# Batch 0 of an attention and MLP kernel: wide value products, six chunks prepared at once, fillers and Fourier tiles in another order, buffers on 128 bytes

## The chip, the cores and the metric

The kernel runs on one NeuronCore of a Trainium2 chip. The metric is the time of one execution on the device in microseconds (us). Instructions run on five engines, each with its own in-order queue: PE (TensorE, matmuls; PEld is its weight load), DVE (VectorE), ACT (ScalarE), POOL (GpSimd) and SP, which issues most DMAs. The engines wait for each other by semaphores only.

## What is computed

Four batches go through linear attention with a decaying state, then a Fourier mixing block with an MLP, then a token mixing block with an MLP. All is float32; products that need it are made of three fp32r matmuls on high and low parts (`three`).

```python
# attention: B=4, H=8, S=768, D=48
for t in range(S):
    state = alpha[:, :, t, :, None] * state + einsum('bhd,bhe->bhde', k[:, :, t], v[:, :, t])
    y[:, :, t] = einsum('bhd,bhde->bhe', q[:, :, t], state)
x = y of all heads side by side            # 4 x 768 x 384
# first block
u = x + real(fft(fft(x, axis=1), axis=2))
un = (u - mean(u)) / sqrt(var(u) + 1e-6)   # over the 384
x = u + relu(un @ w_ch1) @ w_ch2           # 384 -> 1536 -> 384
# second block
u = x + token_mlp(x)                       # over the 768 tokens, 256 wide
out = u + relu(u @ w2_ch1) @ w2_ch2
```

## The kernel before

**Attention in visits.** Two heads make a unit; a unit has six chunks of 128 tokens, so a batch has 4 units and 24 visits (`STEPS`), one for each chunk k. PE's part of visit k (`visit` under `block.tensor`): the scores of chunk k+1 (`attn_scores`, L1313; the two heads lie on rows 0 to 47 and 64 to 111), keys times values of chunk k+1 (`attn_kv`, L1326, needs `krt` from ACT), the value products of chunk k (`attn_back`, L1335: `at` of one head is the stationary operand and that head's 48 columns of `vt` stream), the product with the decayed state (L1340, 96 columns, not for the first chunk of a unit), and the transpose of the keys of chunk k+2 (`attn_turn`, L1306). An fp32 matmul shows as two instructions in the trace, so the two value products are x4 there. DVE masks the scores (`at`, L977), adds up the state (`st`), and prepares the chunks' decay products by scans (`piece_suffix`, `piece_prefix`, three chunks in one piece in batch 0); POOL multiplies them into keys and queries (`prep_k`, `prep_q`) and decays one head's state (`dec`); ACT copies `krt`, `x`, the other `dec`, and in some visits tests the range of the decays (`tested`, L658) or makes a weight's high part (`weight_hi`, at the visits in `HI_AT`; POOL's low parts, `weight_lo`, are at `LOW_AT`).

**Batch 0 has no MLP beside it.** Its 24 visits run first and alone; the visits of batches 1 to 3 are laid between the MLP matmuls of the batch before (the slots h of `VISIT`). After the visits comes the tail of slots h = 31 to 47 (`tail` on each engine, an order written by hand): fold and flips, the six Fourier tiles `f1` (L1299 to L1301 by way of `three`, each wants the low part `xl` of its tile from DVE, and its result is split to `gh` by ACT and `gl` by DVE), the second Fourier products `f2_v`, `f2_u`, `f2_middle`, their sums on DVE and POOL, the normalisation, three transposes (`norm`), and then the first MLP stage. For batch 0 `fill(n)` puts n matmuls on constants, whose result nobody reads, behind the visits and behind the slots named in `FILL`.

**The first MLP slots.** DVE's last slot of the tail (h = 47) reduces the range of the next batch's first unit (`extreme`, L826) and prepares its first chunk (`prep`), and then comes the rest of the normalisation of batch 0 (`norm_stats`, L1081, `norm_var`, `norm_scale`), on which ACT's `std` and `norm_rows` wait, and behind them in ACT's queue the copy `qz` for the first scores of batch 1 (L1317).

**Loads.** SP loads the units in order; POOL issues the four table loads in visits 3 to 6. Buffers lie one behind the other from byte 16512 (a multiple of 128); by this `hh` and `hl`, the stationary operands of the second MLP product, begin 64 bytes past a multiple of 128, `nh`, `nl`, `u2h` and `u2l`, the streamed operands of the first, at a multiple.

## Time and profile before

| | |
|---|---|
| median of 3 runs | 927.83 us (927.74 to 928.92) |
| the profiled execution | 927.87 us, its span 926.1 us |
| PE busy | 904.9 us, 98% |
| DVE, ACT, POOL busy | 49%, 33%, 22% |
| batch 0: visits, then tail up to the first MLP matmul | to 71.0 us, to 98.9 us |
| last long wait of PE ends | 107.58 us |

The page gives busy time as the share of the span, and a line PEclk with the clock that TensorE was granted in 40 slices of 23 us, in tenths of 2.4 GHz (5 is 1.2 GHz). Views of the trace give the same by stretches, and the instructions in order of time.

### The profile page before, as it was taken

The numbers are of one execution on the slowest core, as the hardware profiler recorded it, in microseconds if no ns is written. First come the engines' busy times: TensorE is split into PE (matmuls) and PEld (weight loads), VectorE is DVE, ScalarE is ACT, GpSimd is POOL, SyncE is SP. The second block draws the span as 40 slices with busy tenths as digits, with TensorE's granted clock in tenths as the row PEclk, the third lists the DMA queues.
The fourth block names the chain that finished last, engine by engine and source line by source line (L and its number), as shares of the span: only waits on it lengthen the run. The fifth ranks groups of instructions, "written<-read, shape, count | busy, mean of one in ns | idle before, by whom it ended". The sixth has DMA issues, their size and how long they took to land.

```text
span 926.1 us, 14520 instructions
## 1 busy us (share of the span) xinstructions
PE 904.9 (98%) x5378; PEld 871.6 (94%) x5378; DVE 451.8 (49%) x1078; ACT 303.7 (33%) x794; POOL 201.4 (22%) x330
## 2 busy tenths in 40 slices
PE   8999799999999999999999999999999999999998
PEld 6888699999899998999999999999999999999998
DVE  5446777756877658777472226221422232223121
ACT  3445445432555424444323333211122122112111
POOL 4443463302333103333013332000200020002000
PEclk8559899999999999999999999999999999999999
DMA  9802122004031040220017102000200020000000
GB/s 272 323 1 76 41 60 58 27 6 111 27 86 32 27 116 26 60 58 27 2 69 230 52 3 95 6 26 1 76 0 25 0 76 0 25 10 16 0 25 26
DMA packets 14360, 50.87 MB, mean 55 GB/s; under 512 B 1408, under 2 KB 5632, under 8 KB 12368
## 3 DMA queue, kind: packets, MB, share of 16 engines
q1 hardware_dynamic: 13728, 47.01, 16.3%
q0 software_dynamic: 576, 3.15, 0.9%
q8 instruction: 31, 0.51, 0.2%
q14 instruction: 25, 0.20, 0.1%
HBM read 40.72 MB, written 9.44 MB: 54 GB/s over the span
## 4 chain that ended last, share of the span: by engine, by line
PE 90%; DVE 5%; ACT 2%; DMA 1%; issue 1%; SPq 0%; DVEq 0%; ACTq 0%
PE bank L1299 13%; PE bank L1301 13%; PE bank L1300 13%; PE pair L1299 11%; PE pair L1300 11%; PE pair L1301 11%; PE bank L1335 5%; PE pair L1317 4%; PE bank L1340 3%; PE pair L1326 2%; PE pair L1313 2%; DMA vt<-v 1%; PE bank L1306 1%; PE bank L1434 1%; DVE stats L1081 1%
## 5 line engine op out<-in xcount | busy, mean ns | idle before, releaser
L1168 DVE SCALAR_TENSOR_TENSOR hl<-bank,hh 128x384 fp32r<-128x384 f32 x192 | 106.9, 557 | 333.5 <-ACT hh L742 333.5
L742 ACT ACTIVATE hh<-bank 128x384 fp32r<-128x384 f32 x192 | 94.2, 491 | 353.2 <-PE bank L1301 353.0
L1299 PE MATMUL bank<-nh,w1h 128*128 128x384 f32 x288 | 102.3, 355 | 0.4 <-DVE nl L1124 0.4
L1299 PE MATMUL pair<-w2h,hh 128*128 128x384 f32 x288 | 101.6, 353 | 0.0
L1299 PE MATMUL bank<-u2h,w3h 128*128 128x384 f32 x288 | 97.2, 338 | 0.8 <-DVE u2l L1255 0.8
L1299 PE MATMUL pair<-w4h,hh 128*128 128x384 f32 x288 | 98.0, 340 | 0.0
L1300 PE MATMUL pair<-w4l,hh 128*128 128x384 f32 x288 | 97.3, 338 | 0.0
L1301 PE MATMUL bank<-nh,w1l 128*128 128x384 f32 x288 | 97.3, 338 | 0.0
L1301 PE MATMUL pair<-w4h,hl 128*128 128x384 f32 x288 | 97.2, 338 | 0.0
L1300 PE MATMUL bank<-nl,w1h 128*128 128x384 f32 x288 | 97.1, 337 | 0.0
L1300 PE MATMUL pair<-w2l,hh 128*128 128x384 f32 x288 | 97.0, 337 | 0.0
L1301 PE MATMUL pair<-w2h,hl 128*128 128x384 f32 x288 | 97.0, 337 | 0.0
L1301 PE MATMUL bank<-u2h,w3l 128*128 128x384 f32 x288 | 96.6, 335 | 0.0
L1300 PE MATMUL bank<-u2l,w3h 128*128 128x384 f32 x288 | 96.4, 335 | 0.0
L608 POOL TENSOR_TENSOR u<-u,x2l 128x384 f32<-128x384 f32 x24 | 23.6, 1012 | 276.7 <-DVE u L1276 276.7
L525 POOL TENSOR_TENSOR qkap<-qkap,suf 112x128 f32<-112x128 f32 (+1 forms) x81 | 39.8, 491 | 134.5 <-DVE suf L850 121.0
L977 DVE TENSOR_TENSOR at<-pair,mask 128x256 f32<-128x256 f32 x96 | 40.1, 417 | 52.1 <-PE pair L1326 44.1
L1335 PE MATMUL bank<-vt,at 128*128 128x48 f32 x384 | 63.8, 295 | 0.0
L1335 PEld LDWEIGHTS bank<-vt,at 128*128 128x128 f32 x384 | 61.1, 223 | 1.6 <-issue 0.9
L632 ACT ACTIVATE qz<-qkap 48x128 f32<-48x128 f32 x144 | 44.3, 308 | 40.5 <-POOL qkap L533 34.1
L1299 PEld LDWEIGHTS bank<-nh,w1h 128*128 128x128 f32 x288 | 54.8, 190 | 1.4 <-issue 0.8
L1299 PEld LDWEIGHTS bank<-u2h,w3h 128*128 128x128 f32 x288 | 54.1, 188 | 2.1 <-issue 2.1
(189 smaller groups left out, 1886.3 us busy)
## 6 DMA issues: line engine op xcount, KB each, us to landing
qkap<-qka SPq DMA_DIRECT2D x15, 1011.5 KB, 6.5
vt<-v SPq DMA_DIRECT2D x16, 288.0 KB, 7.8
raw_a<-w_ch SPq DMA_DIRECT2D x6, 768.0 KB, 9.1
mid<-u SPq DMA_DIRECT2D x8, 576.0 KB, 2.8
raw_b<-w_ch SPq DMA_DIRECT2D x6, 768.0 KB, 6.0
out<-u SPq DMA_DIRECT2D x8, 576.0 KB, 2.8
xr<-mid SPq DMA_DIRECT2D x7, 576.0 KB, 3.9
raw_t<-w_tok SPq DMA_DIRECT2D x2, 768.0 KB, 5.5
```

The costliest lines, as they stand in the source:

```text
L525: pool.tensor_tensor(keys.rearrange("p (c n) -> p c n", n=P), keys.rearrange("p (c n) -> p c n", n=P), after.rearrange("p (c n) -> p c n", ...
L608: pool.tensor_tensor(u2[:, t, :], u2[:, t, :], x2l[:, t, :].bitcast(F32), ALU.add).then_inc(s_u2, 1)
L632: act.activation(qz[head_rows(h), k % 2, h, :], q_of(a, k, head_rows(h)), ACT.Copy).then_inc(s_qz, 1)
L742: act.activation(hh[:, s % 4, :], bank[s % 2][:, 0:HALF], ACT.Relu).then_inc(s_hhi, 1)
L977: dve.tensor_tensor(at[:, k % 2, :, :], scores, mask[:, None, :].to_broadcast([P, 2, P]), ALU.mult).then_inc(s_at, 1)
L1168: dve.scalar_tensor_tensor(out=hl[:, s % 4, :], in0=bank[s % 2][:, 0:HALF], scalar=0.0, in1=hh[:, s % 4, :].bitcast(F32), op0=ALU.max, op1 ...
L1299: pe.matmul(out_ap, wh, rh, start=first, stop=False)
L1300: pe.matmul(out_ap, wh, rl, start=False, stop=False)
L1301: return pe.matmul(out_ap, wl, rh, start=False, stop=last)
L1317: return pe.matmul(score_bank(a, k)[:, 0:2 * P], k_of(a, k), qz[0:PR, k % 2, :, :].rearrange("p h t -> p (h t)"), start=True, stop=True)
L1335: mm = pe.matmul(y[:, h * D:(h + 1) * D], at[:, k % 2, h, :], vb[:, c, h * D:(h + 1) * D], start=h == 0, stop=c == 0 and h == 1)
L1340: mm = pe.matmul(y, q_of(a, k), dec[0:PR, k % 3, :], start=False, stop=True)
```

## The change

**Value products.** For batch 0 each of the two value products of a visit streams all 96 columns of `vt` (both heads) and writes two groups of 48 columns: the head's own into `y`, which now begins at column 64, and the other head's, of no use, 112 columns away, into columns that nobody reads.

**Preparation.** DVE and POOL prepare chunks 1 to 5 in the visit -2, where chunks 3 to 5 had been spread over the visits -1 and 0.

**Orders.** Fillers: 2 in place of 4 behind the visits, none at slots 31 and 45. The Fourier tiles of the second part run as 1, 2, 0 (`f1_tile`), and `f2_v(0)` waits for five split tiles in place of six, `f2_u(0)` for the sixth. POOL issues the tables in visits 7 to 10; high and low weight parts come two and three visits later; `weight_lo` 7 goes from the end of the tail into batch 1's visits. The early sums of the fold move to the last two visits, in all batches. DVE prepares the next batch's first chunk in slots 45 and 46, between the splits of the normalised tiles, instead of slot 47; the third of these tiles is transposed into another bank and waits no more for the first's split.

**Buffers.** Two sizes are rounded up and three places moved to 128 bytes. By the offsets `hh` and `hl` go from 64 past a multiple of 128 to a multiple (so do `krt`, `at` and `qz`), `nh`, `nl`, `u2h`, `u2l` and `un` from a multiple to 64 past it.

```diff
+ASIDE = 112
...
-KV_AT, T_AT = 384, 256
+KV_AT, T_AT, Y_AT = 384, 256, 64
...
-FILL = {31: 5, 42: 3, 44: 2, 45: 1, 46: 2}
-HI_AT = (9, 11, 13, 15, 17, 19)
+FILL = {42: 3, 44: 2, 46: 2}
+TABLES_AT = 7
+HI_AT = (11, 13, 15, 17, 19, 21)
 HI_FOLD = 9
-LOW_AT = (12, 15, 18)
+LOW_AT = (15, 18, 21)
 LOW_F1 = 6
-LATE_LOW_AT = (0, 2, 4, 6)
+LATE_LOW_AT = (-2, 0, 2, 4, 6)
...
+NEXT_AT = 45
...
+def f1_tile(i):
+    return i % KT if i < KT else (i + 1) % KT
...
+    def aligned(n):
+        return -(-n // P) * P
+    QB = aligned(QW * 4)
...
+    o = aligned(o)
     suf = sb("suf", [P, 2, 3 * HW + 5], o); o += 2 * (3 * HW + 5) * 4
-    krt = sb("krt", [P, 2, PR], o); o += 2 * PR * 4
+    o = aligned(o)
+    krt = sb("krt", [P, 2, P], o); o += 2 * P * 4
...
-    o += 2 * QB
-    o_u = o
+    o = o_u = aligned(o + 2 * QB)
...
-    NORM_BANKS = (6, 7, 6, 6, 6, 6)
+    def norm_bank(b, t):
+        return bank[4 if b == 0 and t == 2 else 7 if t == 1 else 6]
...
-        return visit_bank(a, k)[:, 0:PW]
+        first = 0 if a else Y_AT
+        return visit_bank(a, k)[:, first:first + PW]
...
-                    prep_k(0, 1, 2)
-                    prep_q(0, 1, 2)
-                elif k == -1:
-                    prep_k(0, 3, 3)
-                elif k == 0:
-                    prep_q(0, 3, 3)
+                    for first, n in ((1, 2), (3, 3)):
+                        prep_k(0, first, n)
+                        prep_q(0, first, n)
                 elif k % 3 == 1 and k + 5 < STEPS:
                     prep_k(0, k + 5, 3)
-                elif k % 3 == 2 and k + 4 < STEPS:
+                elif k % 3 == 2 and 0 < k < STEPS - 4:
...
-                if 3 <= k < 7:
-                    pool.dma_start(tables[k - 3][0][:], tables[k - 3][1].bitcast(F32R)).then_inc(s_table, 16)
+                if TABLES_AT <= k < TABLES_AT + 4:
+                    table, source = tables[k - TABLES_AT]
+                    pool.dma_start(table[:], source.bitcast(F32R)).then_inc(s_table, 16)
...
-                if a == 0:
-                    pool.wait_ge(s_un[0], 2)
-                    for i in range(LOW_F1, 2 * NA - len(LATE_LOW_AT)):
-                        weight_lo(i)
                 if a + 1 < B:
-                    prep(a + 1, 0)
+                    prep_k(a + 1, 0, 1)
+                    if a == 0:
+                        weight_lo(LOW_F1)
+                    prep_q(a + 1, 0, 1)
...
-                    piece_suffix(1)
-                    piece_prefix(1)
-                elif k == -1:
-                    piece_suffix(2)
-                elif k == 0:
-                    piece_prefix(2)
-                elif k % 3 == 1 and k + 5 < STEPS:
+                    for i in (1, 2):
+                        piece_suffix(i)
+                        piece_prefix(i)
+                elif k % 3 == 1 and k > 0 and k + 5 < STEPS:
                     piece_suffix(piece_of(k + 5))
-                elif k % 3 == 2 and k + 4 < STEPS:
+                elif k % 3 == 2 and 0 < k < STEPS - 4:
...
-                if k in (FLAG + 2, FLAG + 3):
-                    early_sum(a, k - FLAG - 2)
+                if k in (STEPS - 2, STEPS - 1):
+                    early_sum(a, k - STEPS + 2)
...
+                if h == NEXT_AT and a + 1 < B:
+                    prep_suffix(a + 1, 0)
+                    prep_inverse(a + 1, 0)
+                if h == NEXT_AT + 1 and a + 1 < B:
+                    extreme(a + 1, 0, 0)
                 for t in NORM_AT.get(h, ()):
                     norm_split(a, t)
+                if h == NEXT_AT + 1 and a + 1 < B:
+                    extreme(a + 1, 0, 1)
+                    prep_prefix(a + 1, 0)
                 if h == 46:
                     for i in range(2):
                         fourier_u(a, 4, 2, i)
-                if h == SLOTS - 1 and a + 1 < B:
-                    for i in range(2):
-                        extreme(a + 1, 0, i)
-                    prep(a + 1, 0)
...
+                    if a:
+                        mm = pe.matmul(y[:, h * D:(h + 1) * D], at[:, k % 2, h, :], vb[:, c, h * D:(h + 1) * D],
+                                       start=h == 0, stop=c == 0 and h == 1)
+                    else:
+                        first = Y_AT * (1 - h)
+                        both = visit_bank(0, k)[:, first:first + 2 * ASIDE].rearrange("p (g n) -> p g n", g=2)[:, :, 0:D]
+                        mm = pe.matmul(both, at[:, k % 2, h, :], vb[:, c, :], start=h == 0, stop=c == 0 and h == 1)
...
-                    pe.wait_ge(s_glo, (a + 1) * (2 * KT))
+                    pe.wait_ge(s_glo, a * (2 * KT) + 2 * KT - 1)
...
-                if j == 1:
+                if j == 0:
+                    pe.wait_ge(s_glo, (a + 1) * (2 * KT))
+                elif j == 1:
...
-                elif t == 2:
+                elif t == 2 and b:
                     pe.wait_ge(s_nlo, b * NC + 1)
-                else:
+                elif t > 2:
...
-            fill(4)
+            fill(2)
```

On PE, the visits of chunks 2 and 3 of batch 0 (`at` the masked scores, `vt` the values, `dec` the decayed state, `krt` the turned keys). Before:

```order
L1313 MATMUL pair1<-qkap0_57 128x128 x2
L1326 MATMUL pair1<-vt0_62,krt_70 112x96
L1335 MATMUL bank6<-vt0_62,at_71 128x48 x2
L1340 MATMUL bank6<-dec_74,qkap0_57 128x96
L1306 MATMUL bank6<-ident_97,qkap0_57 128x112
```

Now:

```order
L1330 MATMUL pair1<-qkap0_57 128x128 x2
L1343 MATMUL pair1<-vt0_62,krt_70 112x96
L1358 MATMUL bank6<-vt0_62,at_71 128x2x48 x2
L1362 MATMUL bank6<-dec_74,qkap0_57 128x96
L1323 MATMUL bank6<-ident_97,qkap0_57 128x112
```

Nothing moves here; the third row streams 2x48 columns where it streamed 48.

On PE, the end of batch 0's visits and the start of its tail (`mask`, `ident` are the fillers, `x`, `flip` the flips, `dfth` the first Fourier tile). Before:

```order
L1335 MATMUL bank7<-vt3_93,at_71 128x48 x2
L1340 MATMUL bank7<-dec_74,qkap3_84 128x96
L1487 MATMUL bank0<-mask_96,ident_97 128x256 x4
L1379 MATMUL pair0<-x_64,flip_98 128x384 x2
L1379 MATMUL pair1<-x_64,flip_98 128x384
L1487 MATMUL bank0<-mask_96,ident_97 128x256 x5
L1299 MATMUL pair1<-dfth_53,xh_61 128x194
```

Now:

```order
L1358 MATMUL bank7<-vt3_93,at_71 128x2x48 x2
L1362 MATMUL bank7<-dec_74,qkap3_84 128x96
L1511 MATMUL bank0<-mask_96,ident_97 128x256 x2
L1401 MATMUL pair0<-x_64,flip_98 128x384 x2
L1401 MATMUL pair1<-x_64,flip_98 128x384
L1316 MATMUL pair1<-dfth_53,xh_61 128x194
```

Two fillers ahead of the flips and all five between the flips and the first tile are gone.

On DVE, slots 43 to 47 of batch 0's tail and what follows (`un` normalised rows, `nl` their low parts, `ext`, `suf`, `inv` and the last `qkap0` the next batch's first unit, `stats` the rest of the normalisation). Before:

```order
L1118 TENSOR_SCALAR un_77<-u0_89,mv_103,nrm_104 128x384 x2
L1124 TENSOR_TENSOR nl_86<-bank6,nh_85 128x3x128
L1124 TENSOR_TENSOR nl_86<-bank7,nh_85 128x3x128
L1124 TENSOR_TENSOR nl_86<-bank6,nh_85 128x3x128
L1067 TENSOR_TENSOR u0_89<-u0_89,pair1 128x2x193
L1067 TENSOR_TENSOR u0_89<-u0_89,pair1 128x2x191
L826 TENSOR_REDUCE ext_105<-qkap0_57 112x1 x2
L850 SCALAR_TENSOR_TENSOR suf_69<-qkap0_57,zeros_99 112x128
L856 RECIPROCAL inv_75<-suf_69 112x1
L862 SCALAR_TENSOR_TENSOR qkap0_57<-qkap0_57,inv_75,zeros_99 112x128
L1081 BN_STATS stats_102<-u0_89 128x6 x3
```

Now:

```order
L1131 TENSOR_SCALAR un_77<-u0_89,mv_103,nrm_104 128x384 x2
L865 SCALAR_TENSOR_TENSOR suf_69<-qkap0_57,zeros_99 112x128
L871 RECIPROCAL inv_75<-suf_69 112x1
L1137 TENSOR_TENSOR nl_86<-bank6,nh_85 128x3x128
L1137 TENSOR_TENSOR nl_86<-bank7,nh_85 128x3x128
L839 TENSOR_REDUCE ext_105<-qkap0_57 112x1
L1137 TENSOR_TENSOR nl_86<-pair1,nh_85 128x3x128
L839 TENSOR_REDUCE ext_105<-qkap0_57 112x1
L877 SCALAR_TENSOR_TENSOR qkap0_57<-qkap0_57,inv_75,zeros_99 112x128
L1080 TENSOR_TENSOR u0_89<-u0_89,pair1 128x2x193
L1080 TENSOR_TENSOR u0_89<-u0_89,pair1 128x2x191
```

The two reductions, the two scans and the reciprocal stood between the last sum of `u0` and `stats`; they stand ahead of that sum now, two of them ahead of the splits `nl`.

## Rows read from the trace of the kernel before

**Rows 1.** The page: the span, and the clock granted in 40 slices.

```profile
span 926.1 us, 14520 instructions
PEclk8559899999999999999999999999999999999999
```

**Rows 2.** Stretches: length, busy time (instructions) of each engine, granted clock, DMA share, GB/s.

```profile
14.00:16.00 2.00, 1.21 (x9) 1.04 (x10) 1.20 (x2) 1.89 (x6) 1.31 (x3) 0.92 1.00 306
...
72.00:74.00 2.00, 2.00 (x7) 1.61 (x6) 2.00 (x6) 1.90 (x4) 0.00 (x0) 0.58 0.06 16
...
110.00:112.00 2.00, 2.00 (x9) 1.97 (x9) 0.85 (x3) 0.25 (x2) 1.29 (x3) 0.69 0.00 0
```

**Rows 3.** In order of time: start, us, engine, line, count, idle before and releaser.

```profile
14.06 0.94 ACT L658 ACTIVATE tested<-qkap,limits 112x768 f32<-112x768 f32 x1 [1.74 <-DMA vt<-v]
...
14.18 0.49 PE L1313 MATMUL pair<-qkap 48*128 48x128 f32 x4 [1.32 <-POOL qkap L533]
...
15.29 0.44 PE L1326 MATMUL pair<-vt,krt 128*112 128x96 f32 x2 [0.61 <-ACT krt L625]
```

**Rows 4.** In order of time, PE: scores that open visits, at either clock.

```profile
9.89 0.49 PE L1313 MATMUL pair<-qkap 48*128 48x128 f32 x4
...
11.20 0.49 PE L1313 MATMUL pair<-qkap 48*128 48x128 f32 x4
...
24.95 0.80 PE L1313 MATMUL pair<-qkap 48*128 48x128 f32 x4
...
27.28 0.80 PE L1313 MATMUL pair<-qkap 48*128 48x128 f32 x4
```

**Rows 5.** In order of time, PE: 48 and 96 columns and the next, at either clock.

```profile
11.89 0.60 PE L1335 MATMUL bank<-vt,at 128*128 128x48 f32 x4
...
12.33 0.43 PE L1340 MATMUL bank<-dec,qkap 112*128 112x96 f32 x2
...
12.60 0.26 PE L1306 MATMUL bank<-ident,qkap 112*128 112x112 f32 x1
...
31.30 0.98 PE L1335 MATMUL bank<-vt,at 128*128 128x48 f32 x4
...
32.09 0.71 PE L1340 MATMUL bank<-dec,qkap 112*128 112x96 f32 x2
...
32.58 0.39 PE L1306 MATMUL bank<-ident,qkap 112*128 112x112 f32 x1
```

**Rows 6.** Stretch of six visits at the lower clock, columns as in rows 2.

```profile
47.91:63.78 15.87, 15.87 (x76) 13.15 (x75) 7.00 (x20) 8.40 (x23) 8.29 (x10) 0.50 0.00 0
```

**Rows 7.** In order of time: fillers, low parts, first Fourier tile, first second-stage product.

```profile
70.98 3.26 PE L1487 MATMUL bank<-mask,ident 128*128 128x256 f32 x8
...
75.13 1.49 DVE L1039 TENSOR_TENSOR xl<-xf,xh 128x384 fp32r<-128x384 f32 x3
...
77.98 0.44 PE L1299 MATMUL pair<-dfth,xh 128*128 128x194 f32 x1
...
86.29 0.36 PE L1299 MATMUL pair<-csh,gh 128*128 128x194 f32 x1 [0.82 <-DVE gl L1044]
```

**Rows 8.** In order of time: DVE's splits and reductions, PE's wait for batch 1.

```profile
96.46 1.06 DVE L1124 TENSOR_TENSOR nl<-bank,nh 128x384 fp32r<-128x384 f32 x2 [0.84 <-ACT nh L715]
...
98.18 0.56 DVE L1124 TENSOR_TENSOR nl<-bank,nh 128x384 fp32r<-128x384 f32 x1 [0.66 <-ACT nh L715]
...
99.58 1.80 DVE L826 TENSOR_REDUCE ext<-qkap 112x1 f32<-112x768 f32 x2
...
107.58 1.22 PE L1317 MATMUL pair<-qz,qkap 112*128 112x256 f32 x2 [4.65 <-ACT qz L632]
```

**Rows 9.** In order of time, PE in the second MLP: either product's first matmuls.

```profile
640.36 0.34 PE L1299 MATMUL bank<-u2h,w3h 128*128 128x384 f32 x1
...
641.92 0.34 PE L1299 MATMUL pair<-w4h,hh 128*128 128x384 f32 x1
...
643.51 0.34 PE L1299 MATMUL bank<-u2h,w3h 128*128 128x384 f32 x1
```

More of the change, by code:

```diff
@@ L100, in program @@
     XB = NC * DM * 4
-    QB = QW * 4
+    def aligned(n):
+        return -(-n // P) * P
+    QB = aligned(QW * 4)
     o_q = o
@@ L369, in f1_out @@
     def f1_out(i):
-        cols = f1_cols(i // KT, i % KT)
+        cols = f1_cols(i // KT, f1_tile(i))
         out_ap = bank[5 + i % 3][:, 0:cols.stop - cols.start]
-        return out_ap.rearrange("p (a n) -> p a n", a=2) if i % KT == 1 else out_ap
+        return out_ap.rearrange("p (a n) -> p a n", a=2) if f1_tile(i) == 1 else out_ap
     def v_terms(a, j):
@@ L624, in attn_krt @@
                     act.wait_ge(s_vis, visited(a, k - 2))
-                    act.activation(krt[:, s % 2, :], turned(a, k), ACT.Copy).then_inc(s_krt, 1)
+                    act.activation(krt[:, s % 2, 0:PR], turned(a, k), ACT.Copy).then_inc(s_krt, 1)
             def attn_qz(a, k, h):
@@ L678, in split_x @@
                 act.wait_ge(s_fold, a * 7 + (4, 7)[part])
-                for t in range(KT):
+                for i in range(part * KT, (part + 1) * KT):
+                    t = f1_tile(i)
                     m = slice(t * P, (t + 1) * P)
@@ L687, in split_g @@
                     act.wait_ge(s_fold, a * 7 + 7)
-                act.activation(g_slot(gh, i // KT, i % KT), f1_out(i), ACT.Copy).then_inc(s_ghi, 1)
+                act.activation(g_slot(gh, i // KT, f1_tile(i)), f1_out(i), ACT.Copy).then_inc(s_ghi, 1)
             def copy_v(a, j):
@@ L715, in norm_split @@
                 act.activation(nh[:, :, t * P:(t + 1) * P],
-                               bank[NORM_BANKS[t]][:, 0:DM].rearrange("p (k n) -> p k n", k=KT), ACT.Copy
+                               norm_bank(b, t)[:, 0:DM].rearrange("p (k n) -> p k n", k=KT), ACT.Copy
                                ).then_inc(s_nhi, 1)
@@ L845, in prep_suffix @@
                 slot, first = suf_at(k)
+                if k % NC == 0:
+                    dve.wait_ge(*unit_loaded(a, k // NC))
                 if k >= RING:
@@ L1035, in split_x @@
             def split_x(a, part):
-                for t in range(KT):
-                    dve.wait_ge(s_xhi, a * 6 + 3 * part + t + 1)
+                for i in range(part * KT, (part + 1) * KT):
+                    t = f1_tile(i)
+                    dve.wait_ge(s_xhi, a * 6 + i + 1)
                     m, r = slice(t * P, (t + 1) * P), slice(part * KT, (part + 1) * KT)
@@ L1043, in split_g @@
                 dve.wait_ge(s_ghi, a * (2 * KT) + i + 1)
-                dve.tensor_tensor(g_slot(gl, i // KT, i % KT), f1_out(i), g_slot(gh, i // KT, i % KT).bitcast(F32),
+                dve.tensor_tensor(g_slot(gl, i // KT, f1_tile(i)), f1_out(i), g_slot(gh, i // KT, f1_tile(i)).bitcast(F32),
                                   ALU.subtract).then_inc(s_glo, 1)
@@ L1123, in norm_split @@
                 cols = slice(t * P, (t + 1) * P)
-                dve.tensor_tensor(nl[:, :, cols], bank[NORM_BANKS[t]][:, 0:DM].rearrange("p (k n) -> p k n", k=KT),
+                dve.tensor_tensor(nl[:, :, cols], norm_bank(b, t)[:, 0:DM].rearrange("p (k n) -> p k n", k=KT),
                                   nh[:, :, cols].bitcast(F32), ALU.subtract).then_inc(s_nlo, 1)
@@ L1325, in attn_kv @@
                 pe.wait_ge(s_krt, s + 1)
-                return pe.matmul(kv_of(a, k), krt[:, s % 2, :], vt[unit_buffer(a, k // NC)][:, k % NC, :], start=True,
+                return pe.matmul(kv_of(a, k), krt[:, s % 2, 0:PR], vt[unit_buffer(a, k // NC)][:, k % NC, :], start=True,
                                  stop=True)
@@ L1334, in attn_back @@
                 for h in range(2):
-                    mm = pe.matmul(y[:, h * D:(h + 1) * D], at[:, k % 2, h, :], vb[:, c, h * D:(h + 1) * D],
-                                   start=h == 0, stop=c == 0 and h == 1)
+                    if a:
[5 more added lines that the diff above has]
+                        mm = pe.matmul(both, at[:, k % 2, h, :], vb[:, c, :], start=h == 0, stop=c == 0 and h == 1)
                 if c:
@@ L1381, in f1 @@
             def f1(a, i):
-                part, t = i // KT, i % KT
+                part, t = i // KT, f1_tile(i)
                 pe.wait_ge(s_xlo, a * 6 + i + 1)
@@ L1433, in norm @@
                 for k in range(KT):
-                    mm = pe.transpose(bank[NORM_BANKS[t]][:, k * P:(k + 1) * P], un[:, t % 3, k * P:(k + 1) * P],
+                    mm = pe.transpose(norm_bank(b, t)[:, k * P:(k + 1) * P], un[:, t % 3, k * P:(k + 1) * P],
                                       ident[:, :])
```

## The prediction

> **What bounds the kernel now.** I read the page first: PE is busy 98% of the span, so on the face of it only PE's work counts. The clock line tells otherwise for the start [rows 1]: 0.5 in two slices of 23 us where everything after is near full. The stretches [rows 2] show when: the clock falls at the end of the slice 14 to 16, in which PE had little to do, and comes back in the slice 72 to 74. In between lie the visits of batch 0: PE is never idle there and runs at 1.2 GHz. Such "busy" time is not work that must take so long. Two visits of the same make (first chunk of a unit, no state product) give the ratio: 9.89 to 11.20 at 2.4 GHz, 24.95 to 27.28 at 1.2 GHz, 1.31 against 2.33 us, 0.562 [rows 4]. What the engine did ahead of the two returns: a run of 256-column fillers from 70.98 on [rows 7], and MLP matmuls in the slice 110 to 112, which shows 0.69 [rows 2]. Ahead of the fall: waits [rows 3]. The change can win in three places: the visits (15.3 to 71.0), the tail up to batch 1's first scores (71.0 to 107.6), and the rate of the matmuls themselves.
>
> My sum is made against the profiled execution, 927.87 us (span 926.1 and 1.8 around it); the median of the runs is 927.83, so nothing is to be converted. About 0.2% (1.9 us) is what a measurement of this kernel can tell from no change.
>
> **Six chunks at once: nothing by itself.** PE's wait for POOL's queries at 14.18 (1.32 us) goes [rows 3]. But what is late next is the same event: ACT's range test of unit 1 stands in visit 0 as before, waits for unit 1's load until 14.06, takes 0.94, and `krt` behind it lets PE go on at 15.29 [rows 3]. SP's order, and so the landing, is untouched. PE then does the scores of chunk 3 early and waits some 1.9 us for `krt` in place of 1.3 and 0.6. The scans that DVE now does ahead of the first `at`, and POOL's two products ahead of the first `dec`, lie in time in which both waited for PE; 0 each, at most 0.3. I expect the clock to fall here again.
>
> **Wide value products: the term that decides.** Each of the four instructions of a visit streams 96 columns in place of 48, which makes a visit more like the stretches before the two returns. If the clock comes back in the visits, each visit after that shrinks. What the columns cost: four 48-column instructions take 11.89 to 12.33, 0.11 each, two of 96 columns 12.33 to 12.60, 0.135 each; at the lower level 31.30 to 32.09, 0.197, and 32.09 to 32.58, 0.245 [rows 5]. So +0.10 us a visit at the higher level and +0.19 at the lower; ends 0 (the weight load hides it) and the price of the rival D below. The Trainium skill (TensorE: Matmul & The Clock Gate, Part 2, "LDWEIGHTS") makes a load of 128 columns take 107 ns whatever is streamed, which the 0.11 agrees with and the 0.135 does not; by it the wide products would be free and the forecast about 2 us lower.
>
> Remaining visits: 22 value products from 15.3 to 71.0, 55.7 us, 2.53 each. At the higher level 2.53 x 0.562 = 1.42, +0.10 = 1.52. The other engines don't shrink with PE: six visits take 7.00 us of DVE, 8.40 of ACT, 8.29 of POOL [rows 6], 1.17, 1.40 and 1.38 a visit. All fit, but ACT's 0.94 of a range test [rows 3] comes in one piece in 8 visits and keeps `krt` waiting; 8 x 0.94 / 22 = 0.34 at most, 0 at least; I take 0.13, since ACT idles in most visits. So 1.65 a visit, 0.652 of now (1.52 to 1.86). At the lower level 2.72, 1.075 of now.
>
> When does the clock return? No row shows it for such visits. The fillers that begin at 70.98 brought it back before 74 [rows 2, 7]; I allow about twice that, 7 us at the lower level after 15.3. Then 7 / 1.075 = 6.5 of the 55.7 us are done, 49.2 x 0.652 = 32.1 are left, the visits end at 54.4: **-16.6**. Ends inside this case: no fall at all and 1.52 a visit, -22.2; 1.86 a visit, -12.5.
>
> **Loads and weight parts: 0.** Tables two to four visits later, high and low parts two and three visits later: with shorter visits these come at about the clock times of now or before the flips, which wait for the tables. The low part that moves into batch 1 is needed by the first second-stage product of the MLP, several us later.
>
> **Fillers and Fourier tiles: -2.8.** The low parts of the first tile are done at 75.13 + 1.49 / 3 = 75.6, yet the first Fourier matmul runs at 77.98, behind the five fillers [rows 7]: 2.3 us. The order 1, 2, 0 and the earlier start of `f2_v(0)` take the wait of 0.82 before it away [rows 7], since the last tile runs while the one before is split. DVE's queue between them gives back some 0.3. What is late next is the same chain through `gl`, only earlier. If a missing filler lets the clock fall in the tail, up to 2 us come back.
>
> **Next batch's preparation: -1.2.** DVE's reductions (1.80) with scans and reciprocal stand between the last split and the rest of the normalisation, on which ACT's `qz` and so PE's wait of 4.65 hang [rows 8]. Moved forward, they fill DVE's waits of 0.84 and 0.66 for ACT [rows 8], 1.5 us; one reduction ahead of the third split holds the first MLP matmul up by 0.3. Queued behind them are only the sums of `u0`, which come later anyway. The early sums, now in the last two visits, have DVE's free time there: 0, at most +0.3.
>
> **Buffers: -3.0.** In the second MLP nine matmuls with `w3h` as weights take 640.36 to 641.92, 0.1733 each, nine with `hh` 641.92 to 643.51, 0.1767 [rows 9]. `hh` and `hl` begin 64 bytes off and are aligned now. There are 6 x 288 = 1728 such matmuls in both MLPs: 5.7 us if the offset is all of it, 0 if it is something else; and as `nh` and `u2h` move the other way, the same 5.7 could be lost on the streamed side. I take -3.0, nearer to the gain, as the row shows the weight side only.
>
> **Sum:** -16.6 - 2.8 - 1.2 - 3.0 = -23.6; 927.87 - 23.6 = 904.3, say **904**.
>
> **The rivals.**
>
> A, the forecast: the clock returns early in the visits and stays. 904; ends -22.2 - 5 - 5.7 and -12.5 - 2.8, so 895 to 912.
>
> B, it returns halfway or falls again at a wait. With a return at 43 us: 27.7 / 1.075 = 25.8 done, 29.9 x 0.652 = 19.5 left, end 62.5, -8.5; with -7.0 of the rest, 912 (909 to 918). For it: no stretch with visits alone, in 55 us, brought the clock back.
>
> C, the change doesn't do what it adds columns for: the visits stay at 1.2 GHz. 55.7 x 0.075 = +4.2; the tail begins low and without fillers, so the flips and the first tile lose about 1.3 of the gain there: -1.5 - 1.2 - 3.0. 927.87 - 1.5 = 926.4 (923 to 929). For it the same as for B, against it that the fillers, which do nothing but stream more columns, brought it back at once.
>
> D, slower: the product's result is written in two runs of 48 columns with a gap, and the write, not the weight load, sets its pace. Place: L1335, at the lower level. Price: twice the spacing, 0.197 x 4 = 0.79 a visit, 17.4 us over 22 visits, less 5.7 of the rest, 939.6; it decides from 5.7 / 22 = 0.26 a visit on; in the middle 934 (929 to 940). The rows speak neither way, as no matmul of before writes in two runs. The Trainium skill (Advanced Engine Details and Errata, "PSUM Cachelines") says that a non-contiguous pattern in PSUM slows matmuls significantly; no row here shows it, and here the runs are long.
>
> **How the numbers follow.** A 0.58, B 0.15, C 0.14, D 0.10, and 0.03 for a time below A. The point is A's, 904. The range 896 to 927 holds nearly all of A and B and most of C, some 0.82. Faster by over 0.2% (under 926.0): A, B, the 0.03 and a third of C, 0.81. Within: 0.09 of C. Slower: D, 0.10.
>
> **What would show it.** The clock line: one low slice, not two, and the visits ending near 54 us. If it is up before 25 us, A; if only at 40, B; if at the fillers, C. Value products: spacing of 0.13 at the higher level; 0.2 or more speaks for D. `krt` waits for the range test at 15.3 as now. The first Fourier matmul comes 4.6 us behind the last state product, not 7; `f2_v(0)` without a wait; PE's wait for `qz` near 3.5 us. Matmuls with `hh` at 0.174 and those with `u2h` no slower. The prediction is wrong if the clock falls again after each load or range test, or if ACT holds the visits above 1.9 us.

## The result and the profile after

The changed kernel takes 921.81 us (median of four executions, 921.35 to 922.73), the kernel before beside it 928.04: a ratio of 0.9933 (95%: 0.9915 to 0.995). That is 6 us faster where 24 were forecast. An execution of this kernel has one of two times, by whether the clock holds in batch 0's visits; where a kernel showed both, they are told apart below.

The page after, span and clock:

```profile
span 919.5 us, 14499 instructions
...
PEclk8558999999999999999999999999999999999999
```

Two low slices are there as in [rows 1]. The stretches (columns as in rows 2) date them:

```profile
14.00:16.00 2.00, 0.09 (x1) 0.09 (x1) 0.96 (x1) 1.32 (x4) 0.27 (x1) 1.00 1.00 264
16.00:18.00 2.00, 2.00 (x11) 1.75 (x11) 1.30 (x4) 1.36 (x4) 1.08 (x2) 0.50 0.94 244
72.00:74.00 2.00, 2.00 (x7) 1.64 (x6) 1.52 (x5) 1.73 (x4) 0.00 (x0) 0.50 0.03 8
74.00:76.00 2.00, 2.00 (x6) 0.86 (x5) 2.00 (x7) 1.76 (x4) 0.00 (x0) 1.00 0.03 8
```

PE does almost nothing from 14 to 16, the clock is at 1.2 GHz from 16 on, and the visits never bring it back: it is up again from 74 on, behind the fillers that begin at 72.02, as before. The rows that answer to [rows 3], in order of time, show the wait ahead of the fall in one piece now:

```profile
12.94 0.49 PE L1330 MATMUL pair<-qkap 48*128 48x128 f32 x4
...
14.68 0.94 ACT L670 ACTIVATE tested<-qkap,limits 112x768 f32<-112x768 f32 x1 [2.44 <-DMA vt<-v]
...
15.91 0.65 PE L1343 MATMUL pair<-vt,krt 128*112 128x96 f32 x2 [2.49 <-ACT krt L637]
```

One visit at the lower clock, PE in order of time (for rows 4 and 5; the view ends within the last row, of which only the start is read):

```profile
23.02 0.80 PE L1330 MATMUL pair<-qkap 48*128 48x128 f32 x4
...
24.23 1.06 PE L1358 MATMUL bank<-vt,at 128*128 128x96 f32 x4
25.08 0.63 PE L1362 MATMUL bank<-dec,qkap 112*128 112x96 f32 x2
25.51 0.39 PE L1323 MATMUL bank<-ident,qkap 112*128 112x112 f32 x1
25.84 0.58 PE L1330 MATMUL pair<-qkap 48*128 48x128 f32 x2
```

The tail and the way to batch 1, in order of time (for rows 7 and 8):

```profile
72.02 1.97 PE L1511 MATMUL bank<-mask,ident 128*128 128x256 f32 x4
...
76.78 0.36 PE L1316 MATMUL pair<-dfth,xh 128*128 128x194 f32 x1 [0.78 <-DVE xl L1052]
...
84.32 0.36 PE L1316 MATMUL pair<-csh,gh 128*128 128x194 f32 x1
...
104.31 0.84 PE L1334 MATMUL pair<-qz,qkap 112*128 112x256 f32 x2 [3.83 <-ACT qz L644]
```

With the same rows of before (70.98, 77.98, 86.29, 107.58 and the span) they divide the 6.6 us of the two spans:

| stretch | before | after | difference | forecast |
|---|---|---|---|---|
| start to the fillers behind the visits | 70.98 | 72.02 | +1.0 | -16.6 |
| to the first Fourier tile | 7.00 | 4.76 | -2.2 | -2.3 |
| to the first second-stage product | 8.31 | 7.54 | -0.8 | -0.5 |
| to batch 1's first scores | 21.29 | 19.99 | -1.3 | -1.2 |
| to the end of the span | 818.5 | 815.2 | -3.3 | -3.0 |
| sum | | | -6.6 | -23.6 |

One term is wrong, and it is the one that was to decide. Of its +1.0, 0.6 is the later end of the wait (15.91 for 15.29).

Not all of the last row is the buffers' (their own run is below). From the first matmul of the second block to the end the changed kernel is 2.2 us faster. The other 1.1 lie between batch 1's scores and that block, 450.3 us for 451.4, and are not steady: in a second trace of the changed kernel it is 451.1 there. That the row comes near its forecast is in part luck.

### The profile page after: what moved, and what is told of

Read it like the earlier page. It is cut to its first block, busy times and chain, and to the rows that moved or that the text cites. A ratio compares the mean times of both kernels' runs of the same rounds, so it can differ in the third digit from the quotient of the medians.

```text
span 919.5 us, 14499 instructions
## 1 busy us (share of the span) xinstructions
PE 899.2 (98%) x5362; PEld 866.5 (94%) x5362; DVE 453.9 (49%) x1078; ACT 303.7 (33%) x794; POOL 196.1 (21%) x330
## 4 chain that ended last, share of the span: by engine, by line
PE 89%; DVE 6%; ACT 2%; issue 1%; DMA 1%; SPq 0%; DVEq 0%; ACTq 0%
PE bank L1316 13%; PE bank L1317 13%; PE bank L1318 13%; PE pair L1316 12%; PE pair L1317 11%; PE pair L1318 11%; PE pair L1334 4%; PE bank L1353 3%; PE bank L1362 3%; PE pair L1343 2%; PE bank L1358 2%; PE pair L1330 2%; DMA vt<-v 1%; PE bank L1323 1%; PE bank L1458 1%
## 5 line engine op out<-in xcount | busy, mean ns | idle before, releaser
L620 POOL TENSOR_TENSOR u<-u,x2l 128x384 f32<-128x384 f32 x24 | 23.6, 1016 | 275.0 <-DVE u L1293 275.0
L1317 PEld LDWEIGHTS bank<-nl,w1h 128*128 128x128 f32 x288 | 54.7, 190 | 0.4
L1316 PEld LDWEIGHTS pair<-w2h,hh 128*128 128x128 f32 x288 | 54.4, 189 | 0.2
```

Of the source, the lines that this page charges most:

```text
L620: pool.tensor_tensor(u2[:, t, :], u2[:, t, :], x2l[:, t, :].bitcast(F32), ALU.add).then_inc(s_u2, 1)
L1316: pe.matmul(out_ap, wh, rh, start=first, stop=False)
L1317: pe.matmul(out_ap, wh, rl, start=False, stop=False)
```

## The experiments

All are edits of the changed kernel, unless another is named, and were run beside the kernel before.

### Narrow value products: the columns cost nothing

```diff
-                    if a:
+                    if True:
                         mm = pe.matmul(y[:, h * D:(h + 1) * D], at[:, k % 2, h, :], vb[:, c, h * D:(h + 1) * D],
```

> The changed kernel with the value products of batch 0 narrow again (48 columns, the head's own). Theory 1, the wide columns neither cost nor bring anything, since at the lower clock the weight load sets the pace of 48 and of 96 columns alike: value products again 0.21 apart or a little less (the kernel before has 0.20), visits end at 72.0 give or take 0.5, time 921.8 within 1 us. Theory 2, my forecast's price (0.19 us a visit at the lower clock) is right and something else paid it back: the visits end some 4 us earlier and the time is 918. Theory 3, the wide products help in a way not yet seen: 924 or more.

920.9 us (920.2 to 921.6; ratio 0.9908, 0.9891 to 0.9924), with the same two low slices. A visit at the lower clock and the end of the visits, PE in order of time (the view of the visit ends within its last row):

```profile
22.51 0.80 PE L1330 MATMUL pair<-qkap 48*128 48x128 f32 x4
...
23.72 0.98 PE L1353 MATMUL bank<-vt,at 128*128 128x48 f32 x4
24.50 0.71 PE L1362 MATMUL bank<-dec,qkap 112*128 112x96 f32 x2
25.00 0.39 PE L1323 MATMUL bank<-ident,qkap 112*128 112x112 f32 x1
25.32 0.59 PE L1330 MATMUL pair<-qkap 48*128 48x128 f32 x2
```

```profile
71.35 1.97 PE L1511 MATMUL bank<-mask,ident 128*128 128x256 f32 x4
```

From scores to scores it is 2.81 us, with wide products 2.82. Four narrow products take 0.78 and the two that follow 0.50; four wide ones 0.85 and 0.43: 1.28 either way. From the end of the wait to the fillers it is 55.99 us (15.36 to 71.35), with wide products 56.11 (15.91 to 72.02). Theory 1 holds; at this clock the wide columns neither cost nor bring more than 0.1 us.

### Fillers in the wait: the fall was the wait's

```diff
                     mm = attn_scores(a, k + 1)
+                    if a == 0 and k == 2:
+                        for _ in range(6):
+                            pe.matmul(pairs[(k + 1) % 2][:, 0, P:P + 256], ident[:, :],
+                                      mask[:, None, :].to_broadcast([P, 256 // P, P]), start=True, stop=True)
                     if has_state(k + 1):
```

> The changed kernel with six fp32 fillers of 256 columns on PE in the wait of 2.49 us ahead of the fourth keys-times-values product (13.4 to 15.9), about 0.39 us each, so nothing is added to the path. Theory 1, the wait alone makes the clock fall, and a clock that is up stays up in the visits: no low slice before the tail, 56.1 us of visits shrink to 0.56 to 0.65 of it, the visits end near 50, time 897 to 903. Theory 2, the visits themselves hold too little work for the clock: it falls some us later, the visits end at 66 to 72, time 915 to 922. The fillers cost at most 0.5 if they outlast the wait.

900.9 us (900.05 to 902.6; ratio 0.9694, 0.9676 to 0.9712). The page:

```profile
PEclk9998999999999999999999999999999999999999
```

and PE around the place, in order of time:

```profile
13.30 0.49 PE L1330 MATMUL pair<-qkap 48*128 48x128 f32 x4
13.72 2.86 PE L1378 MATMUL pair<-mask,ident 128*128 128x256 f32 x12
16.41 0.34 PE L1343 MATMUL pair<-vt,krt 128*112 128x96 f32 x2
...
48.99 1.06 PE L1515 MATMUL bank<-mask,ident 128*128 128x256 f32 x4
```

The twelve instructions fill the wait, no low slice is left ahead of the tail, and the visits end at 48.99 instead of 72.02. Six matmuls whose result nobody reads are worth 21 us: theory 1, in this place. A wait alone does not always do it: in the tail of the changed kernel PE waited 1.40 us up to 97.03, and the clock shows 1.00 from 94 to 104.

### The same with narrow products: what the wide ones are good for

The two edits above together. 

> The changed kernel with the six fillers in the wait and with narrow value products, beside the same with wide ones. Theory 1 (the wait alone makes the clock fall): as with wide ones, 896 to 903, the narrow ones 0 to 2 us faster as they stream less. Theory 2, wide products are what keeps a clock that is up from falling: with narrow ones it falls again in the visits, time 912 to 922, while with wide ones it stays up.

901.2, 901.4, 906.1 and 909.8 us. The last is the profiled one; its stretches:

```profile
34.00:36.00 2.00, 1.82 (x16) 1.50 (x15) 1.49 (x3) 1.93 (x7) 1.44 (x3) 0.89 1.06 407
36.00:38.00 2.00, 2.00 (x12) 1.75 (x11) 1.81 (x5) 1.16 (x3) 1.33 (x2) 0.50 1.03 390
```

With PE busy 1.8 of 2.0 us the clock fell at about 35.6 all the same. Just ahead PE waited twice for `krt`, 0.21 and 0.18 us (up to 33.70 and 35.50); the wide kernel has the same two waits, 0.22 and 0.18, and does not fall. The result is between the theories: narrow visits hold the clock in some executions only.

### Fillers in batch 1's first wait too

```diff
+                    if a == 1 and k == -1:
+                        for _ in range(10):
+                            pe.matmul(bank[5][:, 0:2 * P], ident[:, :], mask[:, None, :].to_broadcast([P, 2, P]),
+                                      start=True, stop=True)
                     mm = attn_scores(a, k + 1)
```

With wide products: 

> The six fillers in the first wait, and ten more of 256 columns (0.39 us each at the higher clock) in the wait of 3.83 us for batch 1's first scores, so that the second fall of the clock goes too. What runs at the lower clock there takes 5.2 us (83.2 to 88.4) and should take about 3.1: theory, 2 us less than with the first fillers alone, 898 to 900. Rival: the fillers outlast the wait or the clock falls anyway, 901 to 903.

With narrow ones: 

> Both groups of fillers, with narrow value products. With narrow products two of four runs lay at 901.3 and two at 906 and 910, the profiled one with a clock that fell in the visits at 35.6. Theory, wide products give the visits what they lack to hold the clock in every run: narrow again spread from 899 to 908 with a median above that of wide ones, and the wide ones within 2 us of each other. Rival, that spread was chance: both 898 to 901.

Wide 899.0 us (898.4 to 900.1; ratio 0.9678, 0.9653 to 0.9703), narrow 898.5, 899.3, 905.7 and 905.8. PE in the wide kernel, in order of time:

```profile
80.18 4.49 PE L1377 MATMUL pair<-mask,ident 128*128 128x256 f32 x20
84.52 0.60 PE L1334 MATMUL pair<-qz,qkap 112*128 112x256 f32 x2
```

Batch 1's first scores take 0.60 where they took 1.22 in [rows 8] and in the kernel with the first fillers alone: the second fall is gone, 2 us. And the spread of the narrow kernel comes again: of eight narrow executions four kept the clock through the visits, of eight wide ones all, and of four more below. If the columns made no difference, all four losses would fall among the eight narrow ones of these twenty about once in 70. So the wide columns, which did not raise the clock, help to keep it up; the evidence for that is this count.

### Fillers in the fallen visits

The six fillers in visit 6 (`k == 6`) in place of 2. 

> The changed kernel with the six fillers not in the wait but in visit 6, well after the clock has fallen, where nothing waits for them to pass: at the lower clock they add 4.7 us (0.39 us each doubled). Theory 1, wide visits can't raise the clock but hold it once it is up: low from 16 to about 31, then up to the end of the visits, 17 visits at 1.55 to 1.65 in place of 2.5 to 2.8, visits end at 57 to 61, time 907 to 911. Theory 2, the visits lose it again or the fillers don't raise it: visits end at 72 to 77, time 920 to 927.

905.7 us (two executions, 905.4 and 906.1; ratio 0.9753, 0.972 to 0.9785). Stretches:

```profile
20.00:22.00 2.00, 2.00 (x11) 1.52 (x11) 0.24 (x2) 1.42 (x4) 0.95 (x1) 0.50 1.05 337
...
24.00:26.00 2.00, 2.00 (x7) 1.64 (x6) 0.00 (x0) 1.16 (x3) 0.56 (x1) 0.50 1.00 318
26.00:28.00 2.00, 2.00 (x9) 1.67 (x8) 0.00 (x0) 0.00 (x0) 0.00 (x0) 0.74 0.67 270
28.00:30.00 2.00, 2.00 (x18) 1.71 (x17) 0.85 (x3) 0.73 (x3) 0.40 (x1) 1.00 0.79 221
...
46.00:48.00 2.00, 2.00 (x18) 1.43 (x16) 1.69 (x5) 1.67 (x6) 1.85 (x3) 1.00 0.00 0
```

Wide visits at 1.2 GHz stay there though PE shows 2.00 busy of 2.00 (20 to 22); the clock rises at 27, within the fillers (23.99 to 28.2); the visits behind them hold it. The first wait had no fillers here; it was 0.90 us, and the clock fell behind it, at 16.8. The expectation's theory 1, and 1 to 6 us better than its number.

### The work behind the load one visit later

```diff
-RANGE_AT = {0: (1, 0), 1: (1, 1), ...
+RANGE_AT = {1: (1, 0), 2: (1, 1), ...
...
+                elif k in (2, 3):
+                    (piece_suffix, piece_prefix)[k - 2](3)
```

and the same two visits for POOL's `prep_k` and `prep_q`. 

> The changed kernel without fillers, but with the work that waits for unit 1's load one visit later: ACT's two range tests of unit 1 in the visits 1 and 2, DVE's scans and POOL's products for the chunks 6 to 8 in the visits 2 and 3. The wait of 2.49 us for the fourth krt goes; by the landing of the load (14.68) and the lengths of one test, one scan and one product (0.94, 0.96, 0.95) I expect a wait of some 1.2 us one visit later and one of about 1 us at the scores of chunk 6. Theory 1, it is the length of one wait that makes the clock fall: it stays up, no low slice in the visits, time 899 to 906. Theory 2, waits of this size are enough: it falls between 16 and 22, time 917 to 923. In between (some runs one, some the other): it stands near its limit.

916.9 us (916.4 to 917.5; ratio 0.9871, 0.9845 to 0.9897). PE's wait, and the stretches around it:

```profile
19.01 0.49 PE L1334 MATMUL pair<-qkap 48*128 48x128 f32 x4 [1.16 <-POOL qkap L548]
```

```profile
16.00:18.00 2.00, 1.85 (x16) 1.44 (x14) 1.68 (x5) 1.47 (x5) 1.13 (x3) 1.00 1.05 314
18.00:20.00 2.00, 0.99 (x9) 0.90 (x10) 1.15 (x3) 1.31 (x4) 1.74 (x2) 1.00 0.98 301
20.00:22.00 2.00, 2.00 (x12) 1.52 (x11) 1.54 (x4) 0.88 (x4) 0.82 (x3) 0.52 0.95 267
```

The wait of 2.49 went, one of 1.16 came later, and the clock fell behind that one, in all four executions: theory 2. What it gains, 5 us beside the first set of the changed kernel and 3 beside the second (below), are two to three visits more at the full clock and the shorter wait.

### The other parts undone

The tail of before (fillers 4, 5 and 1; tile order 0, 1, 2; `f2_v(0)` behind all six tiles):

> The changed kernel with the tail of the kernel before: fillers 4 behind the visits and 5 and 1 at the slots 31 and 45, Fourier tiles in the order 0, 1, 2 and the first second-stage product behind all six split tiles. In the changed kernel the first Fourier tile comes 4.76 us and the first second-stage product 12.30 us behind the end of the last state product's start (72.02). My forecast was 2.3 for the fillers and 0.8 less 0.3 for the order: with both undone the first tile comes 2.0 to 2.4 us later, the second stage a further 0.5 to 0.8, time 924.0 to 925.0. Rival: the fillers shorten a low stretch, so that the old ones cost nothing: 922.

The next batch's preparation back in DVE's slot 47:

> The changed kernel with the next batch's preparation on DVE back in slot 47, behind the last sum. Theory, as forecast (1.2 us): PE's wait for batch 1's scores goes from 3.83 to 5.0 to 5.4 us, the three batches that follow lose 0.2 to 0.4 each at the same place, time 923 to 924.3. Rival, the move only puts the wait elsewhere (the third split came 1.40 us late in the changed kernel, 0.40 in the kernel before): the first MLP product comes 0.9 earlier, the scores 0.3 to 0.5 later, time within 0.5 of 921.8.

The chunks 3 to 5 in the visits -1 and 0 again:

> The changed kernel with the chunks 3 to 5 prepared in the visits -1 and 0 again. Theory, nothing by itself, as forecast: PE waits for POOL's queries and then for krt as in the kernel before, up to the same landing of unit 1, the clock falls at about 16, time 921.8 within 0.7. Rival: the wait is then in two pieces with some work between them and the visits end up to 1 us earlier or later.

The old tail: 923.4, 924.7 and 926.1 us, and 900.4, 901.3 and 901.3 in the three other executions. Old preparation: seven executions from 924.0 to 928.6, four from 902.5 to 903.2. Old chunks: 919.3 (919.1 to 922.8), never lower. PE's waits in the profiled executions, all of which lost the clock, are the next three fences. Old tail:

```profile
14.40 0.43 PE L1343 MATMUL pair<-vt,krt 128*112 128x96 f32 x2 [1.38 <-ACT krt L637]
```

Old preparation:

```profile
14.36 0.43 PE L1339 MATMUL pair<-vt,krt 128*112 128x96 f32 x2 [1.46 <-ACT krt L637]
...
104.57 1.22 PE L1330 MATMUL pair<-qz,qkap 112*128 112x256 f32 x2 [6.38 <-ACT qz L644]
```

Old chunks:

```profile
14.82 0.49 PE L1336 MATMUL pair<-qkap 48*128 48x128 f32 x4 [1.33 <-POOL qkap L548]
```

In the old tail the first Fourier tile comes 7.73 us behind the start of the last state product (69.46 to 77.19), in the changed kernel 5.18 (71.60 to 76.78): 2.55 for the fillers. From there to the second stage it is 8.32 against 7.54: 0.78 for the order. The old preparation makes the wait for `qz` 6.38 in place of 3.83, a loss of 2.5, more than I expected; from the second Fourier stage to batch 1's scores it is 22.26 us against 19.99. The old chunks change nothing that the landing of unit 1 doesn't. That landing varies: ACT's first test of unit 1 starts between 13.13 and 15.48 us in the traces here, and PE's wait goes with it. With the same landing (test at 13.13) the visits end at 70.04 with the old chunks, and at 70.03 with the new ones in the kernel with the old preparation. The 919.3 is below the 921.1 to 922.5 that I expected, but so is the second set of the changed kernel (below).

### The buffers alone

The kernel before with the changed sizes and places:

> The kernel before with only the buffers of the change (two sizes rounded up, three places on 128 bytes). Theory 1, the 64 bytes of the stationary operands cost 0.0015 us in each of 1728 matmuls: 3 us less than before, 925, mostly in the second MLP, 2.2 to 2.7 us between its first and its last matmul. Rival, the rate has another cause: 928 within 0.5.

926.1 us (924.9 to 927.8; ratio 0.9961, 0.9942 to 0.9981), span 923.2. From the first matmul of the second block to the end of the span it is 365.0 us; in the kernel before 367.1 (from 558.98), after 364.9 (from 554.59). The row of the kernel with the buffers alone:

```profile
558.18 0.44 PE L1303 MATMUL bank<-x2h,t1h 128*128 128x384 f32 x1
```

So 2.1 of its 2.9 us are there, just under the 2.2 to 2.7 expected. Of the rest, 0.7 stands ahead of batch 1's first scores (106.91 for 107.58), where unit 1's test began 0.7 us earlier (13.34 for 14.06): the buffers' own share is about 2.2.

### Does the changed kernel ever keep the clock?

The changed kernel again, unedited, and with two and four of the six fillers in the wait.

> The changed kernel once more, in more executions. Theory 1, the fall is not certain but a matter of how long unit 1's load keeps PE waiting in that execution (1.4 to 2.6 us in the runs so far): some executions at 898 to 903, the others at 919 to 923, none in between by more than a late fall explains. Theory 2, with its wait the changed kernel loses the clock always: all executions 919 to 924.

> The changed kernel with two fillers (0.8 us) in the wait in place of six; by the loads so far (wait of 1.4 to 2.6 us) 0.6 to 1.8 us of it are left. Theory 1, what is left of the wait decides, run by run: part of the executions at 900 to 903, part at 919 to 923. Theory 2, any dense work in the wait is enough: all at 900 to 903. Theory 3, only a filled wait is: all at 919 to 923.

> The changed kernel with four fillers (1.6 us); 0 to 1.0 us of the wait is left. Theory 1, most or all executions at 900 to 903, more of them than with two fillers. Theory 2, all. Theory 3, only a wholly filled wait keeps the clock: 919 to 923 wherever anything is left of the wait.

The changed kernel: five executions from 918.9 to 921.3 us, and one of **898.8**. Two fillers: 899.1, 899.7, 900.1 and one of 920.0. Four: 899.5 to 902.9, all four with the clock kept (ratio 0.9693, 0.9678 to 0.9708). What was left of the wait in the profiled executions, changed kernel:

```profile
15.75 0.44 PE L1343 MATMUL pair<-vt,krt 128*112 128x96 f32 x2 [2.07 <-ACT krt L637]
```

Two fillers:

```profile
13.37 1.13 PE L1378 MATMUL pair<-mask,ident 128*128 128x256 f32 x4
15.17 0.43 PE L1343 MATMUL pair<-vt,krt 128*112 128x96 f32 x2 [0.67 <-ACT krt L637]
```

Four:

```profile
13.20 1.99 PE L1378 MATMUL pair<-mask,ident 128*128 128x256 f32 x8
15.71 0.44 PE L1343 MATMUL pair<-vt,krt 128*112 128x96 f32 x2 [0.52 <-ACT krt L637]
```

| wide products, and in the wait | PE's wait in the profiled execution | executions that kept the clock in the visits |
|---|---|---|
| nothing (changed kernel, both sets) | 2.49, 2.07 | 1 of 10 |
| nothing (fillers in visit 6) | 0.90 | 0 of 2 |
| nothing, old chunks | 1.33 | 0 of 4 |
| nothing, work moved | 1.16, later | 0 of 4 |
| nothing, old tail | 1.38 | 3 of 6 |
| nothing, old preparation | 1.46 | 4 of 11 |
| two fillers | 0.67 | 3 of 4 |
| four | 0.52 | 4 of 4 |
| six (three kernels) | 0 | 12 of 12 |

(Counted by the time and the mean granted clock of each execution.) Theory 1 in the first two; four of four fits theory 1 and theory 2 alike. The fall is a matter of chance, and more of the executions keep the clock where little or nothing is left of the wait. In the traces, each wait of 0.90 or more in the visits with nothing in it lost the clock. Its length alone doesn't settle it. The narrow kernel with six fillers (second row, its load the latest) was left with as long a wait as the kernel with the fillers in visit 6 (first row), and kept the clock past it:

```profile
14.72 0.43 PE L1343 MATMUL pair<-vt,krt 128*112 128x96 f32 x2 [0.90 <-ACT krt L637]
```

```profile
16.71 0.43 PE L1343 MATMUL pair<-vt,krt 128*112 128x96 f32 x2 [0.90 <-ACT krt L637]
```

And in the tail five traces, which come there with the clock up, have one and the same wait of 2.05 to 2.06 us ahead of the flips. With six fillers, with four and with two the clock stayed up behind it; with both groups and with the fillers in visit 6 it fell, as the longer flips show. Six fillers, then both groups:

```profile
52.11 2.17 PE L1405 MATMUL pair<-x,flip 128*128 128x384 f32 x6 [2.06 <-DVE tmp L994]
```

```profile
51.28 2.85 PE L1409 MATMUL pair<-x,flip 128*128 128x384 f32 x6 [2.06 <-DVE tmp L994]
```

What tells those executions apart stays open, since only the profiled one of each kernel leaves a trace. That the old tail and the old preparation kept the clock more often than the changed kernel cannot be due to their edits, which stand behind the fall; they were measured on another chip than its second set, with unit 1's test at 13.17 and 13.13 where the changed kernel's two traces have 14.68 and 14.52, and whether that is the reason is not shown. The kernel before, in 44 executions beside all these, never came below 926.6.

### Fillers in the tail's waits as well: the fastest

```diff
-FILL = {42: 3, 44: 2, 46: 2}
+FILL = {31: 2, 42: 3, 44: 4, 46: 5}
...
-            fill(2)
+            fill(7)
```

on top of both groups of fillers. 

> Both groups of fillers and 12 more in the waits of batch 0's tail (five behind the visits, where PE waits 2.06 us for the sums of the fold, two ahead of the first Fourier tile, two and three ahead of the normalised rows and the first MLP product). In one of four runs with both groups the clock fell in the tail at 52.6. Theory, with the waits filled it stays up in every run: 898 to 899, all runs within 1 us. Rival, a filler is late for the work behind it and costs 0.2 to 0.4 each: 899.5 to 901.

898.8 us (898.2 to 899.3; ratio 0.9691, 0.9675 to 0.9708), the clock near full in every slice:

```profile
PEclk9999999999999999999999999999999999999999
```

It is level with 899.0; the fillers there are meant against a fall that the profiled one of those four executions had, and cost nothing. That they prevent it, four executions don't show. Either beats the changed kernel by 21 to 23 us.

## Why the prediction was wrong

**The step that failed** is "7 us at the lower level after 15.3", the return of the clock in the visits. I priced it by the fillers that brought the clock back before 74, and took visits that stream more columns to do the same, only slower. They don't: from 16 to the end of the visits at 72 no wide visit raised it, and the term came out at +1.0 for -16.6. Streaming 96 columns in four instructions of a visit did not do what a run of 256-column matmuls did, and "PE busy" doesn't tell the two apart. I had written the evidence down, under rival B: 55 us of visits had not brought it back. I gave that too little weight.

**The question was put the wrong way round.** I asked whether wide products bring the clock back; what they do, by the counts above, is help to keep it from falling. I even forecast the fall, from the waits in [rows 3], and then looked for what would undo it instead of for what would prevent it. Where the fall was avoided, the lower end of that term held (no fall, 1.52 us a visit, -22.2): with the fillers the visits end at 48.99 against 70.98, and the changed kernel's one lucky execution took 898.8, in case A's lower half. My 1.65 a visit was too high even there: it is 1.48 (16.41 to 48.99 for 22), since the columns cost nothing and the waits behind ACT come to 0.97 in all, 0.04 a visit where I took 0.13.

**Rival C** is what happened, but its price was wrong: +4.2 for the columns, measured 0.1. I read 0.135 and 0.245 in [rows 5] as the cost of 96 columns. In the narrow kernel's visit the product behind four narrow ones pays back what they saved, so that six instructions take 1.28 us whatever they stream. At the higher clock it is the same: in the kernel with fillers in the wait four wide ones take 12.44 to 12.89, 0.45, where four narrow ones took 0.44 [rows 5]:

```profile
12.44 0.61 PE L1358 MATMUL bank<-vt,at 128*128 128x96 f32 x4
12.89 0.39 PE L1362 MATMUL bank<-dec,qkap 112*128 112x96 f32 x2
```

The Trainium skill (TensorE: Matmul & The Clock Gate, Part 2, "LDWEIGHTS") gives the load of 128 columns 107 ns. The 0.11 an instruction at the higher clock agrees with that, wide or narrow; the 0.21 at the lower clock does not. That wide products are free is what I drew from it in the prediction, and it fits these rows where my own reading doesn't. Nor was the 1.3 lost that rival C takes off for a tail that begins low: 2.2 of the fillers' 2.3 came.

**Rival D** didn't occur: two runs of 48 columns with a gap are written at 0.213 us an instruction at the lower clock (four in 0.85), no slower than the 96 columns in one run behind them (two in 0.43). By the Trainium skill (Advanced Engine Details and Errata, "PSUM Cachelines") any non-contiguous pattern slows matmuls significantly; at runs of that length nothing of it shows here.

**Six chunks at once** is as forecast: the landing of unit 1 was late next, 1.9 us forecast, 2.49 and 2.07 measured, and the old chunks showed no gain or loss at the same landing.

**Fillers and Fourier tiles** came out at 2.2 and 0.8 for 2.3 and 0.5, and the old tail gave them back. The 0.82 in front of the second stage is gone, as forecast.

**The next batch's preparation** gave 1.3 for 1.2 in this comparison; undone with the rest of the change in place it costs 2.3 there. Its price came where I put it but was larger: the third split is late by 1.0 for my 0.3 (PE waits 1.40 for it, before 0.40); the wait for `qz` is shorter, 3.83 for 4.65.

**Buffers**: -3.0 forecast, 2.9 by the spans with the buffers alone, of which about 2.2 is theirs. My -3.0 was a choice between two ends, 5.7 and 0, and worked out from nothing. The mechanism is not quite mine: in the second MLP products with `hh` as weights follow each other on average 1.8 ns closer (176.5 to 174.7 ns from start to start, in the traces of before and after) and products with `w3h` 0.6 ns (173.7 to 173.1), so the streamed operands, which moved to 64 bytes past a multiple, lost nothing. Why the second gained is not shown.

**Loads and weight parts**, 0 by the forecast, were not undone alone; the table leaves some tenths for them.

**Sum**: without the visits I had -7.0, measured -7.6. The range held the time by its width: 921.8 lies between the ranges of B (909 to 918) and C (923 to 929), below C's by the price of the columns. The point missed by the one term, which made 70% of the sum.

## What to carry to other kernels

A wait of 1 to 2.5 us on TensorE may cost ten times its length when thin work follows it, as the visits here: look in the clock line for what stands ahead of a low stretch, and prevent the fall there, with matmuls that nobody reads in time that is lost anyway, before looking for a way out of it. Work that did not raise the clock may still hold it: ask the two questions apart. And where a time has two values, four executions on one side don't tell that the other isn't there.

## What the chip showed that I had not expected

- PE at 2.00 busy of 2.00 for 55 us leaves the clock at 1.2 GHz; the run of 256-column fillers that begins at 23.99 in visit 6 has it back at about 27.
- In these visits an fp32 product of 48 columns saves nothing over one of 96, each behind a load of 128 columns: the six instructions take 1.28 us at the lower clock either way.
- The same wait of 2.06 us at the same place of the tail is followed by a fall in some traces (granted clock 0.66 from 52 to 54) and by none in others (1.00).
- One program, one chip, and 898.8 or 921.3 us, with 0.996 and 0.964 as the mean granted clock.
